# Attention probabilities transposed in 32-by-32 blocks by VectorE, values multiplied on eight array tiles, and row sums inverted in threes

## What is computed

```
q_bucket, k_bucket = sign bits of q @ proj, k @ proj        # 6 bits each
mask   = q_bucket[:, None] == k_bucket[None, :]
scores = where(mask, q @ k.T / 8, -1e9);  scores -= max(scores, row)
attn   = exp(scores) / (sum(exp(scores), row) + 1e-9)
x      = attn @ v                     # heads side by side: 1536 x 512
h      = max(x @ w1, x @ w2, x @ w3)  # 512 -> 768
y      = h @ w_out                    # 768 -> 512
out    = gelu-like(y @ w_in) @ w_out2 # 512 -> 2048 -> 512
```

## Time and profile before

| | us |
|---|---|
| median of 3 runs | 671.94 (671.91 to 671.98) |
| span of the profiled execution | 670.8 |
| attention, first instruction to the first product of the layers | 0 to 228.1 |
| TensorE busy, share of the span | 663.7, 99% |
| VectorE, ScalarE, GpSimd busy | 495.9, 346.6, 474.2 |

### The profile page before, as it was taken

The page is one execution under the profiler, slowest core; times in us unless marked ns, Lnnn a source line. Parts: engine busy times, 40 slices in busy tenths (PEclk is TensorE's granted clock), DMA queues, the critical chain, the costliest instruction groups (busy, mean ns, idle before and its releaser), DMA issues.

```text
span 670.8 us, 11966 instructions
## 1 busy us (share of the span) xinstructions
PE 663.7 (99%) x3892; PEld 576.8 (86%) x3892; DVE 495.9 (74%) x976; ACT 346.6 (52%) x761; POOL 474.2 (71%) x538
## 2 busy tenths in 40 slices
PE   8999999999999999999999999999999999999998
PEld 6776777777777699999999999988898988989896
DVE  6878878788788799869778963678877666555554
ACT  6887777877777630011103453555545554454433
POOL 6774756788876899968870528799987776777710
PEclk9999999999999999999999999999999999999999
DMA  6673836638352111111110201212232124212102
GB/s 159 152 161 102 192 88 155 151 88 187 91 132 75 34 32 32 32 32 33 32 40 25 95 1 33 79 48 80 79 93 64 64 78 143 64 64 65 45 18 94
DMA packets 58492, 54.17 MB, mean 81 GB/s; under 512 B 28640, under 2 KB 47488, under 8 KB 58432
## 3 DMA queue, kind: packets, MB, share of 16 engines
q1 hardware_dynamic: 56784, 53.02, 29.2%
q10 hardware_dynamic: 1648, 0.39, 0.3%
HBM read 32.51 MB, written 3.15 MB: 53 GB/s over the span
## 4 chain that ended last, share of the span: by engine, by line
PE 88%; POOL 6%; issue 2%; ACT 1%; DVE 1%; DMA 1%; DVEq 0%; ACTq 0%; POOLq 0%
PE psO L1544 10%; PE psS L1522 10%; PE psR L1530 9%; PE psR L1628 7%; PE psR L1627 7%; PE psR L1629 7%; PE psS L1627 6%; PE psS L1628 6%; PE psS L1629 6%; PE psS L1730 4%; PE psS L1729 4%; PE psS L1728 4%; POOL w_lo L736 3%; PE psR L1470 1%; POOL w_raw L727 1%
## 5 line engine op out<-in xcount | busy, mean ns | idle before, releaser
L577 POOL TENSOR_SCALAR probs<-probs,lone,inv 128x768 f32<-128x768 f32 x96 | 93.9, 985 | 58.6 <-DVE inv L1145 58.5
L736 POOL TENSOR_TENSOR w_lo<-w_raw,w_hi 128x256 fp32r<-128x256 f32 x96 | 79.2, 838 | 44.6 <-ACT w_hi L982 43.9
L1128 DVE TENSOR_REDUCE neg_max<-psS 128x1 f32<-128x768 f32 x96 | 91.2, 950 | 12.9 <-PE psS L1522 8.7
L803 ACT ACTIVATE probs<-psS,neg_max 128x768 f32<-128x768 f32 x96 | 86.5, 901 | 15.7 <-DVE neg_max L1128 15.6
L560 POOL TENSOR_SCALAR w_hi<-w_raw 128x256 fp32r<-128x256 f32 (+1 forms) x79 | 49.0, 624 | 50.2 <-PE psS L1629 28.9
L812 ACT ACTIVATE probs_t<-psR 128x384 f32<-128x384 f32 x131 | 60.7, 491 | 31.2 <-PE psR L1530 30.7
L1530 PE MATMUL psR<-ident,probs 128*128 128x128 f32 x576 | 74.6, 273 | 0.4 <-POOL probs L577 0.2
L1530 PEld LDWEIGHTS psR<-ident,probs 128*128 128x128 f32 x576 | 66.5, 140 | 5.5 <-POOL probs L577 2.1
L1544 PE MATMUL psO<-probs_t,v_raw 128*64 128x384 f32 x384 | 68.8, 494 | 0.0
L1379 DVE TENSOR_TENSOR v_raw<-psR,early 128x384 f32<-128x384 f32 x64 | 35.3, 552 | 32.4 <-PE psR L1629 32.2
L1384 DVE TENSOR_TENSOR v_raw<-v_raw,bits 128x384 f32<-128x384 f32 x64 | 53.7, 841 | 6.7 <-ACT bits L1005 4.3
(11 more groups left out here) (275 smaller groups left out, 1881.5 us busy)
## 6 DMA issues: line engine op xcount, KB each, us to landing
w_raw<-in_moe_w_in SPq DMA_DIRECT2D x16, 512.0 KB, 3.4
w_raw<-in_moe_w_out SPq DMA_DIRECT2D x32, 256.0 KB, 2.7
w_raw<-in_moe_w SPq DMA_DIRECT2D x9, 512.0 KB, 3.8
h_lo<-w_hi SPq DMA_DIRECT2D x22, 192.0 KB, 3.3
h_hi<-w_hi SPq DMA_DIRECT2D x18, 192.0 KB, 3.4
w_raw<-in_q SPq DMA_DIRECT2D x16, 192.0 KB, 3.6
v_raw<-in_v SPq DMA_DIRECT2D x16, 192.0 KB, 2.5
stacks<-w_hi SPq DMA_DIRECT2D x16, 192.0 KB, 3.3
```

Source lines behind the costliest of these rows:

```text
L577: pool.tensor_scalar(probs[i % PROBS][:, :], probs[i % PROBS][:, :], lone[:, i % 6:i % 6 + 1], inv[:, i % 6:i % 6 + 1], ALU.add, ALU.mult) ...
L736: pool.tensor_tensor(in2_slot(w_lo, n, which), in2_raw(n, PARTS2[which]), f32(in2_slot(w_hi, n, which)), ALU.subtract).then_inc(in2_split, 1)
L803: act.activation(probs[i % PROBS][:, :].rearrange("p (a b) -> p a b", a=2), psS[i % 2][:, :, 0:HALF], ACT.Exp, bias=neg_max[:, i % 6:i % 6 ...
L1128: dve.tensor_reduce(neg_max[:, i % 6:i % 6 + 1], psS[i % 2][:, :, 0:HALF], AX.XY, ALU.min).then_inc(max_ready, 1)
```

## The change

The probabilities are no longer transposed on TensorE. `turn_probs` is now one VectorE transpose of 128 x 768 that turns each 32 x 32 block in place of its partition quadrant. Key row r of block b thus lies on partition r of every quadrant, and the quadrant g holds query rows 32g to 32g+31. `times_values` therefore takes 32 keys at a time: a weight tile is 32 rows by 64 columns, the moving operand 96 columns, and eight such products (two heads by four quadrants) lie on the eight tiles of the array and write four banks. One call of `times_values` has 48 of them, and a unit has four calls (`CHUNKS`) in place of six. Since every quadrant needs the values on its own 32 partitions, each value chunk is loaded four times, by four DMAs of 32 partitions.

The ring of banks is gone: `psO` has four banks, which q/k transposes, bit projections and units share by explicit waits. `invert_sums` takes three tiles at a time, with one guard and one reciprocal; the two lone-row results come from two ScalarE activations (`lone_shares`). `probs` has five buffers. SyncE's order is written anew, with 32 value loads at the end of each pair's list and the first 32 ahead of `load_qk(4)`.

```
-                for a in range(2):
-                    sync.dma_start(v_raw[p % 2][a][:, :, :], v_r[2 * p + a, :, :, :]).then_inc(v_loaded[p % 2], 16)
+            def load_v(p, c):
+                if p > 0:
+                    sync.wait_ge(*unit_values(2 * p - 1, c))
                 for a in range(2):
+                    for g in range(QUADRANTS):
+                        sync.dma_start(values[c][a][ts(g, 32), :], v_r[2 * p + a, c, :, :]).then_inc(v_loaded[c], 16)
...
-            load_v(0)
-            load_v(1)
...
+            for c in range(CHUNKS):
+                load_v(0, c)
+            load_qk(4)
+            load_qk(5)
+            place_hi(2)
+            place_lo(2)
+            place_hi(3)
+            place_marks(2)
+            place_marks(3)
+            place_lo(3)
+            for p in range(PAIRS - 1):
+                if p + 2 < PAIRS:
+                    for m in (2 * p + 6, 2 * p + 7):
+                        if m < HEADS:
+                            load_qk(m)
+                    for m in (2 * p + 4, 2 * p + 5):
+                        place_hi(m)
+                        place_lo(m)
+                    for m in (2 * p + 4, 2 * p + 5):
                         place_marks(m)
+                else:
+                    for k in range(3):
+                        load_block(k)
+                for c in range(CHUNKS):
+                    load_v(p + 1, c)
...
+            def lone_shares(i):
+                cols = slice(i % 6, i % 6 + BATCH)
+                for o, bias, scale in ((lone, lone_bias[:, 0:1], 1.0), (lone_sums, lone_bias[:, 1:2], float(S))):
+                    act.activation(o[:, cols], neg_max[:, cols], ACT.Relu, bias=bias, scale=scale).then_inc(lone_found, 1)
...
-            def copy_turned(i, j):
+            def turn_probs(i):
                 u, s = i // NT, i % NT
-                dve.wait_ge(*filled(("probs", i, j)))
+                dve.wait_ge(probs_normed, i + 1)
                 if u >= 2:
-                    dve.wait_ge(unit_out, u - 1)
+                    dve.wait_ge(*unit_values(u - 2, CHUNKS - 1))
+                dve.transpose(probs_t[u % 2][:, s // TH, :, ts(s % TH, 32)],
+                              probs[i % PROBS][:, :].rearrange("p (b r) -> p b r", r=32)).then_inc(probs_turned, 1)
...
-                for a in range(2):
-                    mm = pe.matmul(psO[a * D:(a + 1) * D, 0:HALF], v_raw[p % 2][a][:, c, :],
-                                   probs_t[u % 2][:, a, c, :], start=c == 0, stop=c == NT - 1)
+                if u % 2 == 0:
+                    pe.wait_ge(v_loaded[c], 16 * 2 * QUADRANTS * (p + 1))
+                for t in range(NT):
+                    for a in range(2):
+                        for g in range(QUADRANTS):
+                            mm = pe.matmul(psO[a * D:(a + 1) * D, g, 0:UNIT_COLS], values[c][a][ts(g, 32), ts(t, D)],
+                                           probs_t[u % 2][ts(g, 32), a, CHUNKS * t + c, :],
+                                           start=c == 0 and t == 0, stop=c == CHUNKS - 1 and t == NT - 1)
+                mm.then_inc(values_used, 1)
...
+            for i in range(1, TILES + 2):
+                p, st = i // 12, i % 12
+                if i + 1 < TILES:
+                    scores(i + 1)
...
+                if i >= FIRST_VALUES and (i - FIRST_VALUES) % 6 < CHUNKS:
+                    times_values((i - FIRST_VALUES) // 6, (i - FIRST_VALUES) % 6)
...
+                if st == 8 and p + 2 < PAIRS:
+                    turn_qk(2 * p + 4)
+                    turn_qk(2 * p + 5)
```

More of the change, by code:

```diff
@@ L253, in lsh_attention_ffn @@
         qk_loaded = [sem(f"qk_loaded{i}") for i in range(2)]
-        v_loaded = [sem(f"v_loaded{i}") for i in range(2)]
-        ring_filled = sem("ring_filled")
-        ring_emptied = [sem(f"ring_emptied{i}") for i in range(RING)]
+        v_loaded = [sem(f"v_loaded{i}") for i in range(CHUNKS)]
+        qk_turned = sem("qk_turned")
+        qk_copied = sem("qk_copied")
+        projected = sem("projected")
+        bits_made = sem("bits_made")
         act_stacked = sem("act_stacked")
@@ L562, in make_qk_hi @@
             def make_qk_hi(m):
-                for j in range(2):
-                    pool.wait_ge(*emptied(("turn", m, j)))
+                pool.wait_ge(*copied(m, 1))
                 if m >= 4:
@@ L1140, in invert_sums @@
                 dve.wait_ge(lone_found, 2 * inverted(i))
-                for c in range(i % 6, i % 6 + count):
-                    dve.tensor_scalar(guarded[:, c:c + 1], sums[:, c:c + 1], 1e-9, lone_sums[:, c:c + 1], ALU.add,
-                                      ALU.add).then_inc(sums_guarded, 1)
-                dve.wait_ge(sums_guarded, i + count)
+                dve.scalar_tensor_tensor(guarded[:, cols], sums[:, cols], 1e-9, lone_sums[:, cols], ALU.add,
+                                         ALU.add).then_inc(sums_guarded, 1)
@@ L1200, in _ @@
             row_max(1)
-            invert_sums(0, 1)
             dve.wait_ge(act_stacked, 4)
@@ L1484, in first_project @@
                 pe.wait_ge(proj_signed, 4)
-                o = ring_bank(("bits", 0, a))
+                o = bits_bank(a)
                 for g in range(4):
                     first = MARKS * (g // 2)
-                    mm = pe.matmul(o[ts(g, 32), 0:HALF], proj_block[:, first:first + 32], half(qk_t[a], g % 2), start=True, stop=True,
+                    mm = pe.matmul(o[ts(g, 32), :], proj_block[:, first:first + 32], half(qk_t[a], g % 2), start=True, stop=True,
                                    tile_position=(0, 32 * g))
-                mm.then_inc(ring_filled, 1)
+                mm.then_inc(projected, 1)
             def project(p):
-                for a in range(2):
-                    for j in range(2):
-                        pe.wait_ge(*emptied(("turn", 2 * p + a, j)))
-                o = ring_bank(("bits", p))
+                pe.wait_ge(*copied(2 * p + 1, 1))
+                if p >= 2:
+                    pe.wait_ge(x_lo_made, 2 * p - 3)
+                o = bits_bank(p + 1)
                 for a in range(2):
@@ L1649, in _ @@
                 plain(0, o)
-            for c in range(NT):
+            for c in range(CHUNKS):
                 times_values(UNITS - 1, c)
```

411 lines of the change are left out of this document (135 added, 276 removed).

## The result

The changed kernel takes **754.96 us** (median of 4 runs, 752.73 to 758.15) where the kernel before takes 671.96 beside it: 1.124 times as long, 95% interval 1.121 to 1.127. The forecast was 708.3, within 668 to 765. So the direction and the range held, but the kernel lost 83.0 us where 36.4 were forecast. The profiled execution was the slowest of the four (758.15 us); it has a span of 756.3 us, 85.5 more than before.

The account below looks back on a forecast made before the run. The prediction took TensorE to bound the kernel before and SyncE's DMA queue, 32.5 us a pair, the changed one. The span, 670.8 + 36.4 = 707.2, plus 1.1 for the median gave 708.3 us, range 668 to 765.

Parts of the forecast that it names:

- waits for `in_v` in even units: Expected sign in the attention stage: TensorE's longest waits are for value DMAs, in calls of even units only.
- VectorE's transpose: VectorE in attention: 0.9 us for each 128 x 768 transpose, within a step of 2.05 us a tile, 24.6 a pair.
- ScalarE and GpSimd: Attention stage: ScalarE loses 131 copies and gains two small activations for three tiles, GpSimd is unchanged; both at nothing.
- the queue's sum: SyncE's DMA issues in attention: 32.5 us a pair as the bound, 708 us in all, range 691 to 745, chance 0.60.
- rival 2: TensorE in the values calls can't be fed; harm from a call of 2.24 us, mostly 715 to 765 us; chance 0.15.
- step 85: TensorE's step that needs the fourth value chunk of pair 6, forecast to land at 238.4 us.
- the last pair: End of attention, from 238.4 us: VectorE's steps reach step 97 at 263.0, unit 14 ends at 264.1.
- unit 15: Last unit of values calls: forecast 0.4 us longer, by the start and end of its four calls.
- Part 4: SyncE's queue in attention: 32 value loads a pair at 0.475 us, 15.2, plus 17.3 for other DMAs, 32.5 us a pair.
- Part 1: TensorE in attention: 72 transposes go, -7.9 us a pair; a values call takes 1.05 us; 19.5 us a pair.
- Rival 1: SyncE's queue isn't the bound, as 32-partition loads issue in half the time, 0.23 us or less; 652 us; chance 0.12.
- Rival 3: VectorE's transpose runs at half rate, 1.7 us, 34.2 us a pair; 722 us; chance 0.10.

Follow-up runs that it names:

- the two other bounds out of the way: Changed kernel with both reductions: only quadrant 0's value loads after the first pair (8 a pair) and 24 in place of 48 products a call; 676.9 us.
- half of the products: Changed kernel with 24 in place of 48 products in each values call, SyncE's list of 32 value loads a pair untouched; 727.19 us.
- 8 loads: Changed kernel with only quadrant 0's value loads issued after the first pair, 8 a pair in place of 32; 732.27 us.
- the table of four times: Changed kernel with 32 or 8 value loads a pair: 755.0 and 732.3 us at 48 products a call, 727.2 and 676.9 at 24.
- 16 loads: Changed kernel with both heads of a pair in one DMA per quadrant and chunk, 16 value loads a pair, same bytes and result; 723.23 us.
- 162 products a unit: Kernel before with each values product from the second key chunk on cut into 16 products of 24 columns, 162 in place of 12 a unit; 772.99 us.

## Why the forecast was wrong

**Right.** That the kernel loses, by SyncE's queue, and where it is felt: no pause in the list, waits for `in_v` in even units. VectorE's transpose (0.9 from its start to the next instruction's, as forecast) and its step: with the two other bounds out of the way it fills its windows at 2.05 us a tile, and the time is 677. ScalarE and GpSimd came at nothing. What lies behind the attention went over unchanged: it took 434.3 us from unit 15's end before and 756.3 - 320.9 = 435.4 after.

That 755 lies inside 668 to 765 is no success of the queue's sum, whose own range ended at 745; the margin above that was there for rival 2. By the profiled spans the sum misses 49.1 us (85.5 less 36.4), in four places: 31.0 up to step 85, 12.6 in the last pair, 4.5 in unit 15, and 1.1 behind it.

**The step that failed first is Part 4's price of a value load.** 0.475 us is right for a load that meets nothing: 201 of the 224 loads up to step 85 take 0.426 us each, 0.47 with the gap. The other 23 take 1.48 us on average, each beside a page, and with them a load costs 0.577, gap included: 129.3 us for the 224 where the sum has 106.4, so 22.9 of the 31.0. The placements grew by 7.1, about 1 us a pair; a later start and a slower landing make the last 1.0. The price came from the last load of four, which stands alone in the earlier trace rows; all four took 2.70 us, and in the trace before, the second of them took 1.12 us, with a page at 12.12 us beside it. I took the undisturbed price without a reason for leaving that one out. Changing TensorE's instructions changed SyncE's price (with half of the products it was 0.521), and my sum kept the two apart.

**Part 1 is the second.** I made a call from the array's time, 1.05 us, and thought that what feeds TensorE was covered (4 ns an instruction). Neither held. A run of 192 instructions takes 1.44 us, 7.5 ns each, and above that come the stops and the lower clock; the mean of the first 14 units' calls was 2.06 us. The projection's twelve instructions after a wait could not show what a run of 192 takes. Where a call waited for values anyway this will have cost little, but it did cost in the last pair. There the forecast went from 238.4 to 264.1; measured were 269.4 and 307.7, so 12.6 us more. The chain of waits runs over TensorE, ScalarE and VectorE there and over no DMA, and 7.0 us of it are stops in calls. The longest stands in front of one last matmul:

```profile
270.88 1.42 PE L1492 MATMUL psO<-probs_t,v_more 32*64 32x96 f32 x95
275.95 0.29 PE L1492 MATMUL psO<-probs_t,v_more 32*64 32x96 f32 x1 [3.65 <-issue]
```

Unit 15 takes 8.9 us for its four calls, 4.0 before, where the forecast had 0.4 more.

A relieved queue would not have rescued the number either: with 16 or 8 loads the kernel takes 723 to 732 us, more than the 708.3 that I gave to a kernel bound by the queue. **Rival 2** (TensorE can't be fed) thus had the mechanism that lies right behind. My threshold for it, a call of 2.24 us, was just reached at the lower clock and passed in calls with a stop (135.88 to 140.78, 4.9 us), in 16 of the 64 calls; their mean stayed under it. I had treated the rivals as excluding each other. They lay one behind the other, as the table of four times shows. How much of the second bound is the call's own length, how much the stops and how much the clock wasn't separated.

On the floor of 25 ns from matmul to matmul that the Trainium skill gives ("TensorE: Matmul & The Clock Gate", section "Back-to-back issue gap"): by it, an estimate from the page, a call's 96 matmuls take 2.4 us. The trace has 1.44 at full clock, 12.5 ns a matmul on eight tiles, so the rule doesn't hold for this form. In the kernel before with its products cut up, on two tiles with weights of 128 rows, 29 to 30 ns were measured, a little over it.

**The clock** wasn't in the forecast at all. It was 1.00 throughout before, where TensorE was busy without a pause. In the changed kernel, with pauses of up to 3.65 us, it is at 0.77 to 0.98 in the windows from 50 to 300 us, and a call at the lower level takes up to 2.24 instead of 1.44 us, the scores 1.65 instead of 0.97. I can't give it a share of its own, as no run here kept the clock up with the pauses left in.

**Rival 1** (a load of 32 partitions issues in half the time) was wrong by the same rows that spoke against it: 12, 48 and 96 KB all take 0.42 to 0.5 us. **Rival 3** was wrong as well, by the transpose's 0.964.

**What stays open:** whether a page blocks an issue, and why; why some pages stop TensorE and others don't; and what besides the start puts 16 loads ahead of 8. No version found beats the kernel before. The best that computes the whole result, with both heads in one load, is 4.2% faster than the changed kernel and 7.7% slower than the one before.

## What to carry to other kernels

Where a change multiplies small instructions, give each in-order list its own sum (issues on the DMA queue, instructions on TensorE) at the price of a long run, not of a short one, and expect that the two prices can be coupled: here fewer products made SyncE's issues cheaper, and each long issue stood beside a page of instructions. When two edits each bring back a quarter to a third of a loss, try both together before you call either unimportant; one bound lay behind the other. To cut a queue's time, put more bytes in each issue: the price was the same from 12 to 96 KB, as long as the source wasn't repeated.

## What the runs showed of the hardware

- A DMA issue of 32 partitions takes 0.42 us, 0.466 from start to start, for 12, 48 and 96 KB alike. One of 192 KB whose source repeats the same 32 rows for four quadrants ran at 95 to 109 GB/s, and issues of SyncE took up to 3.3 us with it and behind it.
- An issue of SyncE that starts within 0.6 us before or 0.75 us after the begin of an instruction page took 1.4 us on average (34 long issues beside 36 pages in 202 us, none without a page).
- TensorE's matmuls stopped without a wait for anybody, mostly in the middle of a call of small products, and went on 2.2 to 2.9 us after a page began, in all of the changed kernel's 18 such stops. There was one page for about 250 matmuls and weight loads.
- 96 float32 matmuls and 96 weight loads of 32 x 64 on eight tiles take 1.44 us with 96 columns and 1.15 with 24, at full clock. With weights of 128 x 64 on two tiles it was 29 to 30 ns a matmul with 24 or 48 columns.
- In a long run of such calls TensorE had 256 instructions in 3.7 us, half of it stopped; at 384 in 5.79 us, with weights of 128 rows, it ran without a stop.
- In the variant with 8 loads the granted clock was 0.86 to 0.97 with 96 columns and 0.55 to 0.70 with 24 (windows of 50 us). In the kernel before with 162 products a unit, 24 columns and no pauses, it was 1.00.
